# Fused attention and two MLP stages on one core: mask rows made once and copied, small transfers ahead, a fourth output buffer, the row product first in a head

## What is computed

```python
def _attn_ref(q, k, v):                      # 4, 8, 576, 64
    scores = scale * np.matmul(q, k.transpose(0, 1, 3, 2))
    mask = block_i >= block_j                # blocks of 64 tokens
    scores = np.where(mask, scores, -1000000000.0)
    scores = scores - np.max(scores, axis=-1, keepdims=True)
    attn = np.exp(scores)
    attn = attn / (np.sum(attn, axis=-1, keepdims=True) + 1e-09)
    return np.matmul(attn, v)
...
x = _moe_ref(x, **moe_kwargs)                # r * (relu(xk @ w_k)^2 @ w_v)
return _moe2_ref(x=x, **moe2_kwargs)         # p[e] * (relu(x @ w1[e]) @ w2[e])
```

## Time and profile before

| | us |
|---|---|
| median of three runs | 825.7 |
| the three runs | 825.38, 825.70, 829.25 |
| the profiled execution | 830.44 |
| its span, first to last instruction | 828.6 |
| PE busy in the span | 758.7 |
| attention (to the scores of the last head) | 219.1 |
| first MLP | some 277 |
| routing | some 49 |
| experts | some 283 |

### The profile page before, as it was taken

How to read it: one execution, slowest core, us unless ns; L and a number is a source line. 1 busy time by engine, 2 the same in 40 slices (tenths; PEclk the granted TensorE clock), 3 DMA queues, 4 the chain that set the end, 5 groups by cost and what they waited for, 6 DMA issues and landing times.

```text
span 828.6 us, 12920 instructions
## 1 busy us (share of the span) xinstructions
PE 758.7 (92%) x3991; PEld 663.6 (80%) x3992; DVE 497.3 (60%) x787; ACT 350.1 (42%) x651; POOL 162.7 (20%) x181
## 2 busy tenths in 40 slices
PE   1999999999899999999999991599999999999993
PEld 1777787878689999999999990478888888888882
DVE  8688898998488675849484638432212574444261
ACT  2566776768562624344351300241121554334240
POOL 2244454444210000000010000202212212212201
PEclk9999999999999999999999995599999999999997
DMA  4466666544100010010100012487110066241000
GB/s 130 130 191 185 191 192 184 168 144 117 30 9 1 1 39 1 1 39 1 39 1 38 1 39 78 130 288 255 39 37 30 38 230 241 80 187 37 26 13 9
DMA packets 52802, 74.30 MB, mean 90 GB/s; under 512 B 30061, under 2 KB 30221, under 8 KB 52753
## 3 DMA queue, kind: packets, MB, share of 16 engines
q1 hardware_dynamic: 49152, 64.23, 24.2%
q0 software_dynamic: 3600, 9.44, 3.3%
HBM read 65.30 MB, written 10.56 MB: 92 GB/s over the span
## 4 chain that ended last, share of the span: by engine, by line
PE 78%; DVE 10%; DMA 4%; SPq 2%; issue 2%; POOL 1%; ACT 1%; POOLq 0%; DVEq 0%; ACTq 0%
PE ps L664 19%; PE ps L665 19%; PE ps L666 19%; PE ps L615 7%; PE ps L593 3%; PE ps L773 2%; PE ps L594 2%; PE ps L654 2%; PE ps L568 2%; DMA inv<-inv_scratch 2%; DVE hi L1015 1%; DVE sig L1160 1%; DMA we_raw<-w 1%; PE ps L746 1%; PE ps L571 1%
## 5 line engine op out<-in xcount | busy, mean ns | idle before, releaser
L615 PE MATMUL ps<-pT,v_sb 128*128 128x320 f32 (+4 forms) x448 | 116.3, 384 | 0.0
L615 PEld LDWEIGHTS ps<-pT,v_sb 128*128 128x128 f32 (+1 forms) x448 | 78.7, 199 | 20.2 <-issue 8.7
L664 PE MATMUL ps<-we_hi,hT_hi 128*128 x176 | 72.1, 410 | 3.4 <-DVE hT_lo L1340 3.4
L664 PE MATMUL ps<-we_hi,xgT_hi 128*128 x176 | 72.6, 412 | 2.2 <-DVE xgT_lo L1334 2.2
L665 PE MATMUL ps<-we_lo,xgT_hi 128*128 x176 | 70.4, 400 | 0.0
L666 PE MATMUL ps<-we_hi,xgT_lo 128*128 x176 | 70.2, 399 | 0.0
L665 PE MATMUL ps<-we_lo,hT_hi 128*128 x176 | 70.2, 399 | 0.0
L666 PE MATMUL ps<-we_hi,hT_lo 128*128 x176 | 70.0, 398 | 0.0
L965 ACT ACTIVATE hT_hi<-ps 128x1024 fp32r<-128x1024 f32 x22 | 22.6, 1025 | 109.8 <-PE ps L773 109.8
L797 ACT ACTIVATE pT<-ps 128x256 f32<-128x256 f32 (+2 forms) x192 | 63.9, 389 | 11.5 <-PE ps L594 9.6
L993 DVE TENSOR_REDUCE negm<-ps 128x1 fp32r<-128x128 f32 (+3 forms) x128 | 57.5, 482 | 17.7 <-PE ps L568 17.7
(11 more groups left out here) (198 smaller groups left out, 1653.4 us busy)
## 6 DMA issues: line engine op xcount, KB each, us to landing
we_raw<-w SPq DMA_DIRECT2D x12, 2048.0 KB, 9.5
qk_raw<-qkT SPq DMA_DIRECT2D x32, 576.0 KB, 4.1
v_sb<-v SPq DMA_DIRECT2D x32, 160.0 KB, 3.1
inv<-inv_scratch SPq DMA_DIRECT2D x32, 144.0 KB, 3.0
y_scratch<-ytok SPq DMA_DIRECT2D x6, 768.0 KB, 3.4
wm_raw<-w_k SPq DMA_DIRECT2D x8, 256.0 KB, 3.7
wm_raw<-w_v SPq DMA_DIRECT2D x8, 256.0 KB, 3.3
wm_raw<-w_r SPq DMA_DIRECT2D x4, 256.0 KB, 3.6
```

What stands on the lines that cost most here:

```text
L615: last = mm(ps[:, OUTB + half, q0 - 256 * half:q1 - 256 * half], v_sb[0:rows, j % 2, c, cols], pT[0:rows, i % 2, at + q0:at + q1], start=( ...
L664: mm(dst, a_hi, b_hi, start=(k == 0), stop=False)
```

## The change

- The constant rows are set on DVE in buffer 0 alone (L1043 to L1064 of the changed kernel); SP copies them to buffers 1 and 2 (`copy_masks`, 5 rows of 7 KB each), and PE waits for both copies before the maxima of head 1. `aug` is packed closer (1792 columns instead of 1920).
- In SP's iteration, `load_qk` stands behind `load_inv`, `store_inv`, `load_row` and `spread_sums`. v of two heads lies together and comes in one transfer of twice the run length.
- `o_raw` has four buffers. `copy_out(i)` waits for `normalise(i-4)` instead of `normalise(i-3)`.
- POOL does `split_k(i+3)` before `normalise(i-3)`.
- DVE does `split_q_lo(i+3)` between groups 1 and 2, and `invert(i-1)` between groups 2 and 3; both stood behind group 3.
- PE does the row product of head i + 1 in front of the scores of head i, where it stood behind their second piece.
- `ksq`, a buffer of the first MLP, lies where `qk_raw` was, so ACT waits at head 28 until the last q and k have been read.

```diff
@@ -104,20 +104,23 @@
         hi, aug = [None] * NBUF, [None] * NBUF
         for b in (2, 0, 1):
             hi[b] = place("work", f"hi{b}", [P, 2, S], R32)
-            aug[b] = place("work", f"aug{b}", [AUG, 3, CH * P], R32)
-        Q, KEY, QMAX, QLO, KHI = 0, 1, 0, 1, 2
-        v_sb = place("work", "v_sb", [P, 2, CH, 3 * DH])
+            aug[b] = place("work", f"aug{b}", [AUG, 2 * S + CH * P], R32)
+        Q, KEY, QMAX, KHI, QLO = 0, 1, 0, S, 2 * S
+        v_sb = place("work", "v_sb", [P, 2, CH, 4 * DH])
         pT = place("work", "pT", [P, 2, P_AT[CH]])
         negm = place("work", "negm", [P, 2, CH], R32)
         m_rows = place("work", "m_rows", [CH, 2, P], R32)
         eps = place("work", "eps", [P, 2])
-        o_raw = place("work", "o_raw", [P, NBUF, S])
+        NOUT = 4
+        o_raw = place("work", "o_raw", [P, NOUT, S])
         sums = place("work", "sums", [BLK, 2, S // BLK])
         inv = place("work", "inv", [P, S])
...
@@ -314,25 +316,29 @@
             def load_v(j):
 
                 wait(sp, pv_done, 4 * j - 4)
-                for h in range(2):
-                    sp.dma_start(v_sb[:, j % 2, :, 2 * h * DH:(2 * h + 1) * DH],
-                                 v[2 * j + h:2 * j + h + 1].rearrange("a p (c d) -> (a p) c d", d=DH)).then_inc(
-                        v_loaded[j % 2], 16)
+                sp.dma_start(v_sb[:, j % 2, :, DH:3 * DH],
+                             v[j:j + 1].rearrange("a p (c d) -> (a p) c d", d=2 * DH)).then_inc(v_loaded[j % 2], 16)
 
             def load_row(i):
 
                 sp.wait_ge(row_copied, i + 1)
                 wait(sp, scores_t, 5 * (i - NBUF) + 5)
-                sp.wait_ge(aug_set, min(i + 1, NBUF))
-                sp.dma_start(aug[i % NBUF][DH:DH + 1, QLO, :].bitcast(F32),
+                if i == 0:
+                    sp.wait_ge(aug_copied, 16 * (NBUF - 1))
+                sp.dma_start(aug[i % NBUF][DH:DH + 1, QLO:QLO + CH * P].bitcast(F32),
                              m_rows[:, i % 2, :].bitcast(F32)).then_inc(row_loaded[i % 2], 16)
+
+            def copy_masks(b):
+
+                sp.wait_ge(aug_set, 1)
+                sp.dma_start(aug[b][DH:AUG, :].bitcast(F32), aug[0][DH:AUG, :].bitcast(F32)).then_inc(aug_copied, 16)
 
             def spread_sums(i):
 
                 row = (1 - i % 2) * DH
                 sp.wait_ge(o_copied, 2 * i + 2)
                 wait(sp, inv_stored[i % 2], 16 * (i // 2))
-                sp.dma_start(sums[:, i % 2, :], o_raw[row:row + 1, i % NBUF, :]).then_inc(sums_spread[i % 2], 16)
+                sp.dma_start(sums[:, i % 2, :], o_raw[row:row + 1, i % NOUT, :]).then_inc(sums_spread[i % 2], 16)
 
             def store_inv(i):
 
@@ -365,6 +371,8 @@
             load_qk(0)
             load_qk(1)
             load_v(0)
+            for b in range(1, NBUF):
+                copy_masks(b)
             load_qk(2)
             load_row(0)
             load_qk(3)
@@ -377,20 +385,20 @@
                     sp.dma_start(idw[:, a, col:col + GATE], gate_in[a, :, b, :]).then_inc(mu_loaded, 16)
 
             for i in range(SLOTS):
-                if i + 4 < NHEAD:
-                    load_qk(i + 4)
+                if 3 <= i < NHEAD + 3:
+                    load_inv(i - 3)
                 if 2 <= i < NHEAD + 2:
                     store_inv(i - 2)
                 if i + 1 < NHEAD:
                     load_row(i + 1)
                 if 1 <= i < NHEAD + 1:
                     spread_sums(i - 1)
+                if i + 4 < NHEAD:
+                    load_qk(i + 4)
                 if i % 2 == 0 and i + 2 < NHEAD:
                     load_v(i // 2 + 1)
                 if i < WMLP // WLOAD:
                     load_wm(i)
-                if 2 <= i < NHEAD + 2:
-                    load_inv(i - 2)
 
             for s in range(NSTEP):
                 sp.wait_ge(ytok_done, 3 * s + 3)
...
@@ -460,10 +468,10 @@
             pool.wait_ge(pool_set, 3)
 
             for i in range(NHEAD):
+                if i + NBUF < NHEAD:
+                    split_k(i + NBUF)
                 if i >= NBUF:
                     normalise(i - NBUF)
-                if i + NBUF < NHEAD:
-                    split_k(i + NBUF)
             for i in range(NHEAD - NBUF, NHEAD):
                 normalise(i)
 
...
@@ -621,15 +629,13 @@
             pe.wait_ge(aug_set, 1)
             head_max(0, (0, 1, 2, 3))
             head_row(0)
-            pe.wait_ge(aug_set, 2)
+            pe.wait_ge(aug_copied, 16 * (NBUF - 1))
             head_max(1, (0, 1, 2, 3))
-            pe.wait_ge(aug_set, NBUF)
             for i in range(NHEAD):
                 ahead = i + 2 < NHEAD
-                head_scores(i, (0, 1))
                 if i + 1 < NHEAD:
                     head_row(i + 1)
-                head_scores(i, (2,))
+                head_scores(i, (0, 1, 2))
                 if ahead:
                     head_max(i + 2, (0,))
                 head_scores(i, (3, 4))
@@ -814,8 +820,8 @@
                 q0, q1 = ((0, 256), (256, S))[half]
                 act.wait_ge(pv_done, 2 * i + half + 1)
                 if half == 0:
-                    wait(act, norm_done, i - 2)
-                nc.scalar.activation(o_raw[:, i % NBUF, q0:q1], ps[:, OUTB + half, 0:q1 - q0], ACT.Identity,
+                    wait(act, norm_done, i - NOUT + 1)
+                nc.scalar.activation(o_raw[:, i % NOUT, q0:q1], ps[:, OUTB + half, 0:q1 - q0], ACT.Identity,
                                      bias=eps[:, i % 2:i % 2 + 1]).then_inc(o_copied, 1)
 
             def split_wm_hi(i, cols=WPIECE):
...
@@ -873,6 +879,11 @@
                 copy_out(i, 0)
                 if i == 4:
                     act.wait_ge(pool_set, 3)
+                if i == NHEAD - 4:
+                    act.wait_ge(k_split, NHEAD)
+                    act.wait_ge(q_split, NHEAD)
+                    act.wait_ge(hi_cast, NHEAD)
+                    act.wait_ge(tops_cast, NHEAD)
                 if i in (NHEAD - 4, NHEAD - 2):
                     for c in range(2):
                         xm_first(0, 0, c + (i == NHEAD - 2) * 2)
...
@@ -1027,26 +1038,9 @@
                 vec.tensor_tensor(wm_lo[:, piece], wm_raw[:, piece], wm_hi[:, piece].bitcast(F32),
                                   ALU.subtract).then_inc(wm_split, 1)
 
-            def zero_aug(b):
-
-                vec.memset(aug[b][DH:AUG, :, :].bitcast(F32), 0.0).then_inc(aug_zeroed, 1)
-
...
@@ -1054,21 +1048,31 @@
             dve.wait_ge(const_done, 1)
             vec.tensor_copy(ident_r[:, :], ident[:, :])
             vec.tensor_copy(idw[:, 1, PAD:PAD + P], ident[:, :]).then_inc(const_done, 1)
-            zero_aug(1)
-            set_aug(0)
+            dve.wait_ge(aug_made, 3)
+            chunk_of = ident[DH:AUG, DH + 1:AUG]
+            spread = [AUG - DH, CH - 1, BLK]
+
+            def chunks(at):
+
+                return rows[:, at:at + (CH - 1) * P].rearrange("p (c q) -> p c q", c=CH - 1)
+
+            for at in (QMAX, QLO):
+                vec.tensor_copy(chunks(at)[:, :, 0:BLK], chunk_of.unsqueeze(2).to_broadcast(spread))
+            vec.tensor_scalar(chunks(KHI)[:, :, BLK:P], chunk_of.unsqueeze(2).to_broadcast(spread), NEG, None,
+                              ALU.mult).then_inc(aug_masked, 1)
+            dve.wait_ge(aug_masked, 1)
+            vec.memset(aug[0][DH:DH + 1, KHI:KHI + S].bitcast(F32), 1.0).then_inc(aug_set, 1)
+
             cast_hi(0)
             split_q_lo(0)
-            set_aug(1)
             for g in range(4):
                 head_reduce(0, g)
             copy_row(0)
             cast_hi(1)
             split_q_lo(1)
-            zero_aug(2)
-            set_aug(2)
-            cast_hi(2)
             for g in range(4):
                 head_reduce(1, g)
+            cast_hi(2)
             split_q_lo(2)
 
             def sum_xm(s, w, c):
@@ -1102,15 +1106,16 @@
                     cast_hi(i + NBUF)
                 if i + 2 < NHEAD:
                     head_reduce(i + 2, 1)
+                if i + NBUF < NHEAD:
+                    split_q_lo(i + NBUF)
                 if i + 2 < NHEAD:
                     head_reduce(i + 2, 2)
+                if i:
+                    invert(i - 1)
+                if i + 2 < NHEAD:
                     head_reduce(i + 2, 3)
-                if i + NBUF < NHEAD:
-                    split_q_lo(i + NBUF)
                 if WFIRST <= i < NHEAD - 1:
                     split_wm_lo(i - WFIRST, WPIECE if i < NHEAD - 2 else WLAST)
-                if i:
-                    invert(i - 1)
                 if i == NHEAD - 3:
                     dve.wait_ge(k_split, NHEAD)
                     dve.wait_ge(q_split, NHEAD)
```

46 lines of the change are left out of this document (18 added, 28 removed).

## The result

The changed kernel takes 834.1 us (median of 4 runs, 833.5 to 834.5), the kernel before, run beside it on the same chip, 826.3 us (825.4 to 829.3): a ratio of 1.009, 95% interval 1.006 to 1.011. It is slower by 7.8 us; the sum had said 8.5 and the forecast, 837, was 2.9 too high. The profiled execution of after took 834.0 us, its span is 832.0.

What follows compares the result with a forecast made beforehand. PE was taken as the bound, with DVE 0.37 us behind it. Prologue -7.4, loop +15.3 and end +0.6 gave +8.5 us: 838.9 on the profiled execution, 834.2 on the median, forecast 837, range 819 to 850.

Steps and rivals of the forecast that it cites:

- Prologue: Before head 0's first scores: less mask and buffer work on DVE starts them at 14.8 instead of 22.17 us, -7.4.
- rival D: Prologue: the mask copies land as late as 14.8 us, 4 us on top of the forecast, 841; chance 0.03.
- Loop: Heads 1 to 28: POOL holds DVE's remainder of q, so a head takes 6.7 us, 187.6 against 172.3, +15.3.
- slack of 0.64: In each head: the row product stood 0.64 us behind the first scores, so group 3 could be that much later.
- End: Head 31's row product still waits for ACT, and 0.64 us of scores now stand behind that wait: +0.6.
- Sum: Whole kernel: -7.4 + 15.3 + 0.6 = +8.5 us, 838.9 on the profiled execution, 834.2 on the median.
- 4.7 us between profile and median: Kernel before: the profiled execution's excess over the median, likely in part late rows with their slow clock.
- choice of 837: Whole kernel: the middle taken between 838.9 on the profiled execution and 834.2 on the median.
- B: Loop: the remainder of q isn't blocked and takes 0.74 us, a head takes 5.82, total 809.6; chance 0.15.
- C: Loop: unseen slack partly catches the blocked time, a head takes 6.2 to 6.5 us, 824.4, no change; chance 0.12.
- A: Loop: as forecast, and PE's clock falls again and again, at most +12 us, 849, or 843; chance 0.17.
- The fourth output buffer: Loop: ACT waits for a multiplication one head older, which costs nothing as the multiplication also moved back.

Runs made afterwards that it cites:

- second profile of before: The kernel before, unchanged, run and profiled again: 828.3 us, profiled span 823.6 us.
- row_back: The changed kernel with the row product of the next head behind the second piece of scores again: 813.1 us, ratio 0.984.
- q_last: The changed kernel with the remainder of q back behind group 3: 818.5 us, ratio 0.988.
- q_first: The changed kernel with the remainder of q right behind the rounding, ahead of group 1: 816.4 us, ratio 0.984.
- pool_back: The changed kernel with POOL's multiplication ahead of its remainder of k, as before: 848.5 us, ratio 1.023.
- sp_back: `row_back` with SP's issues in the order of before, q and k of head i + 4 first: 814.3 us, ratio 0.987.
- three_out: `row_back` with three output buffers instead of four: 831.0 us, ratio 1.004.
- hi_later: `row_back` with ACT's first two MLP roundings moved from head 29 to head 30, behind its copy out: 810.6 us, ratio 0.983.
- row_back_tail: `row_back` with ACT's copy out at head 29 ahead of the MLP's two roundings: 813.1 us, ratio 0.980.
- q_first_row_back: `row_back` with the remainder of q right behind the rounding, as in `q_first`: 813.8 us, ratio 0.985.

## Why the prediction was right

**Prologue, forecast -7.4, measured -8.2 to the first scores of head 0, -9.1 to those of head 1.** The first scores come at 13.95 instead of the forecast 14.8. The steps were right, and each was forecast a little late: the first reduction starts at 6.47 (forecast 7.0), the row product at 9.18 (9.7), the last maxima of head 1 at 12.27 (13.0), and 1.68 us follow (1.8). The mask copies were no bound, as in the sum, and rival D's late landing didn't occur. The other 0.9 us are the shorter head 0. The sum had no term for it, and rightly: head 0 took 9.35, 9.79 and 8.69 us in three profiles with the old prologue, so 0.9 is no more than the difference between profiles. Against the second profile of before the prologue is -9.6.

**Loop, forecast 6.7 us a head and +15.3, measured 6.60 and +12.5** against the first profile of before, +14.8 against the second. By steps, from the start of a head's scores:

| step | forecast | measured |
|---|---|---|
| rounding starts | 2.13 | 2.06 |
| POOL's remainder of k | 3.1 to 4.5 | 2.99 to 4.40 |
| remainder of q ends | 5.1 | 5.00 |
| its duration | 1.76 | 1.80 |
| group 3 ends | 6.6 | 6.34 |
| row product to scores | 0.07 | 0.21 |
| next scores | 6.7 | 6.60 |
| PE idle in a head | 0.9 | 0.66 |

The mechanism is right step by step. The term that was mis-sized is what follows the remainder: group 3 takes 0.69 where I took 0.75, and with the overlaps between neighbours group 2, the reciprocal and group 3 need 1.34 instead of 1.5. Against that the hand-over from the row product to the scores takes three times what I had. PE's own time in a head was taken as 5.82 and is 5.94, so its wait is shorter than forecast by more than the period is. `row_back` shows the slack of 0.64 that the forecast said was lost, and `q_last` and `q_first` that the remainder's place decides.

**End, forecast +0.6, measured +0.3 to +1.4** (15.67 us from head 29 to head 31 against 15.37 and 14.25). It can't be told more sharply, since before's own two profiles differ by more.

**Sum.** The first profile of before: -9.1 + 12.5 + 0.3, and -0.3 behind attention, is +3.4, the difference of the spans. The second: -9.6 + 14.8 + 1.4 and +1.8 behind attention is +8.4. The medians say +7.8. The 4.7 us between profile and median I had set down "likely in part" to late rows with their slow clock. The second profile, whose span is 5.0 shorter, is 2.2 shorter in the loop, 1.1 at the end of attention and 2.1 in stages that the change doesn't touch, and 0.4 longer in head 0. PE waits longer for late rows in it, 4.2 us against 2.0, so they don't explain the loop's 2.2; what it lacks are the two stretches at half the clock. The choice of 837, between two baselines, was too high by 2.9. That the same sum on the median, 834.2, meets the measured 834.1 so closely is luck: the prologue and the loop were both forecast too slow (by 1.7 and 2.8 against the first profile, by 2.2 and 0.5 against the second), and what makes up for it is the distance of the first profile from the median, or, against the second, the end of attention and stages that the change doesn't touch.

**The rivals.** B and C fell in after: no head has its remainder of q unblocked, none lies between 6.2 and 6.5. B's time, 809.6, is 3.5 below that of `row_back`, where DVE isn't waited for. A didn't occur in after, whose loop runs at 1.00 throughout, though 0.66 us of each head are idle; in `pool_back` it did.

**What was costed at nothing.** SP's order: no effect is shown, and a few us aren't excluded (`sp_back`). The fourth output buffer "costs nothing": right of its cost, and incomplete, for without it POOL's new order costs some 17 us (`three_out`). The new waits of ACT at head 28: ACT waits 0.7 us in after and PE not at all, but PE loses 1.9 us by them in `q_last`, where the remainder of q comes later. The reciprocal ahead of group 3 was costed at its 0.20 us, without a wait of its own: right in after, but in `q_last` and `q_first` its wait for the sums makes group 3 late. Its place wasn't tried by itself either. The pairs of v weren't tried by themselves; PE never waits for v in after.

## What to carry to other kernels

An engine that runs 0.37 us behind the bound has that margin once: two moves that each leave a faster kernel, an earlier reader and a longer chain ahead of it, cost some 21 us together, so add up all edits on one chain before costing any. Of the DVE and POOL operations measured here that overlap, the one that starts first runs at full speed, so order the queues so that the one on the path is first, or put it where the other engine is quiet, and look what else runs there. An instruction put ahead of an urgent one brings its own wait along: a reciprocal of 0.2 us held group 3 back for over 1 us in five heads of `q_last`. A wait in a queue that runs in order doesn't go away when the instruction behind it is put ahead; it goes when the instruction that waits is moved behind all that PE needs (`hi_later` against `row_back_tail`).

## What the runs showed that I had not expected

- A stretch of 3.40 us with 0.66 us idle was followed by half the clock in `pool_back`, and in after, where PE idles 0.66 us in every head, the clock stayed at 1.00 through all 28. What tells the two apart is open.
- In `hi_later` removing one idle stretch of 2.6 us gave 3.8 in the profile, half of it by the clock.
- In `q_last` and `q_first` PE's waits for group 3 come with the reciprocal's wait for the sums, whose transfer is issued late behind the late copy of a row; a held DVE operation that nobody waits for in its own head can cost in the next.
- Heads in which PE shows no idle time differ in length: 5.70 to 5.73 in the first heads of `q_last`, 5.78 to 5.88 in most of `q_first`, some 5.9 in `row_back` and `q_first_row_back`. About 0.1 us goes with the row product's place, and why is open.
